# A sparse-attention and feed-forward kernel: another opening, block means by a selecting matrix, raw weights in the low parts' place

## The chip, the cores and the metric

The kernel runs on one core of one Trainium2 chip. Times are microseconds of device time of one execution, the median of several. One profiled execution gives the trace; there times count from the start of its span.

## The reference, cut to what matters

```python
# q, k, v: (2 batches, 8 heads, 768 positions, 64)
k_sum = k.reshape(B, H, nb, 32, D).max(axis=3)          # block maxima of keys, nb = 24
v_sum = v.reshape(B, H, nb, 32, D).mean(axis=3)         # block means of values
scores_l = scale * q @ k.T, kept where |i - j| < 16, else -1e9
scores_s = scale * q @ k_sum.T + np.log(32)
a = softmax(concatenate([scores_l, scores_s]))
attn = a @ concatenate([v, v_sum])
x = attn as (1536 tokens, 512)
h = maximum(maximum(x @ w1, x @ w2), x @ w3)            # 512 to 768 columns
x = h @ w_out                                           # the feed-forward's result
# then a second mixture of experts: each token with a positive skip score
# passes through one of 8 experts (512 to 1024 to 512) and is added to x
```

## The kernel before, in words

All data is fp32. Products of the feed-forward are made from three fp32r products, of high and low parts: a high part is a rounding copy on ScalarE, a low part is the difference on VectorE. So each weight piece (`w_hi`, `w_lo`) and each block of activations (`x_hi`, `x_lo`, `h_hi`, `h_lo`) is split once.

The kernel has three stretches: attention, the feed-forward, then routing and the experts. The first two are interleaved by an order written out by hand on every engine.

Attention has 24 steps. Step g takes a pair of heads and four tiles of 64 queries. The first twelve steps belong to batch 0 (pairs 0 to 3, each three times, in turn), the others to batch 1. On TensorE a step has three parts: `scores(g)` (windows of 96 keys and 24 block maxima), `turn_probs(g)` (four transposes of the normed probabilities) and `values(g)` (product with the value windows and block means). Between them VectorE scales, masks and takes the maximum (`mask_max`), ScalarE takes four exponentials with row sums (`exps`), VectorE inverts the sums (`invert`), GpSimd multiplies (`norm`), and ScalarE copies the turned probabilities out of PSUM. `x_high` and `x_low` split the result of a step. One PSUM tile holds the scores of one step, and one the values.

Keys of a pair come as `k_all`. VectorE takes the block maxima (`key_max`) and copies windows and maxima into `k_w` (`place_keys`), for all 12 tiles of the pair at once. The block means of values are made on GpSimd from `v_all` by five halving sums (`value_sums`), turned by TensorE (`turn_sums`) and placed by ScalarE (`place_sums`).

The feed-forward has 6 groups of 256 tokens, four steps' results each. A group has 20 units: units 0 to 17 are products of 12 matmuls (six hidden tiles, three weights each), units 18 and 19 are the down products, of 18 matmuls of 512 columns. The maximum over the three weights is taken by a copy on ScalarE (`h_a`) and two maxima on VectorE (`h_m`); `hidden_hi` and `hidden_lo` split it. Three PSUM banks turn among the units. Unit 18 needs hidden tile k at its k-th step of contraction. Between units of the next group, TensorE also transposes the group's result rows and makes logits of them (`tail`).

`step(g)` interleaves: from step 6 on (`FIRST`), five units ride in each step, split in three by `PARTS`. A step on TensorE is scores(g + 2), units, turn_probs(g), units, values(g - 1), units. Units that remain run behind step 23, so group 4 holds the last two attention steps and group 5 none.

The weights are 8 pieces of 768 KB: pieces 0 to 5 hold one hidden tile's three weights, 6 and 7 the down weights. A piece comes into one of two raw buffers (`raw_w`); ScalarE makes the high part and issues the load of the next piece, which waits until VectorE has taken the low part of the piece before. `SPLITS` says in which step which piece is split. All other loads are issued by the SP queue in a fixed order, each behind a wait for its buffer.

## Time and profile before

| | before |
|---|---|
| median of 3 runs | 536.09 us (535.78 to 537.84) |
| the profiled execution | 535.93 us, its span 534.1 us |
| TensorE busy | 465.2 us (87%) |
| VectorE busy | 209.0 us (39%) |
| ScalarE busy | 179.6 us (34%) |
| GpSimd busy | 79.9 us (15%) |
| mean granted TensorE clock | 0.952 of 2.4 GHz |

The shares are averages over the whole span. What an engine does in one stretch is read from the rows by stage, and which wait ends last there from the chain and the timeline.

### The profile page before, as it was taken

How to read it: one execution, taken by the hardware profiler on the slowest of the kernel's cores; microseconds unless marked ns; L12 is line 12 of the kernel's file. 1: busy time of each engine (PE TensorE's matmuls, PEld its weight loads, DVE VectorE, ACT ScalarE, POOL GpSimd, SP SyncE). 2: the span in 40 equal slices, each digit the busy share in tenths (PEclk: the TensorE clock that was granted, in tenths of full speed). 3: DMA queues.
4: the chain of work that ended last, by engine and by line, in shares of the span. 5: the costliest groups of instructions: out<-in, count | busy, mean ns of one | idle time of the engine just before them, and what ended most of it. 6: DMA issues, size and time to landing. Idle time of an engine off the chain costs nothing.

```text
span 534.1 us, 9695 instructions
## 1 busy us (share of the span) xinstructions
PE 465.2 (87%) x3409; PEld 401.6 (75%) x3410; DVE 209.0 (39%) x475; ACT 179.6 (34%) x461; POOL 79.9 (15%) x99
## 2 busy tenths in 40 slices
PE   1557868999999999999999951698999999999974
PEld 1337867899899899999999941476777777787753
DVE  5674457343333323412302237627422222222371
ACT  2585333443433243333111113427222222222360
POOL 2641003322010000010000000011111111111111
PEclk9988879999999999999999975799999999999998
DMA  8747431242130112020020024944611111111000
GB/s 262 254 135 243 139 110 56 56 135 76 29 105 26 39 45 97 16 80 1 14 80 1 2 79 178 360 152 147 216 50 39 39 39 39 39 39 35 22 15 2
DMA packets 20239, 46.64 MB, mean 87 GB/s; under 512 B 3580, under 2 KB 7164, under 8 KB 20208
## 3 DMA queue, kind: packets, MB, share of 16 engines
q1 hardware_dynamic: 16944, 35.25, 19.5%
q0 software_dynamic: 2400, 6.24, 3.5%
q10 hardware_dynamic: 864, 4.72, 2.6%
q8 instruction: 21, 0.34, 0.2%
q14 instruction: 10, 0.08, 0.1%
HBM read 37.86 MB, written 9.96 MB: 90 GB/s over the span
## 4 chain that ended last, share of the span: by engine, by line
PE 77%; DVE 6%; DMA 5%; issue 5%; ACT 3%; SPq 1%; DVEq 1%; POOL 1%; ACTq 0%; POOLq 0%
PE bank L497 29%; PE pair L613 14%; PE bank L603 12%; PE bank L512 9%; PE bank L446 2%; PE pair L416 2%; PE bank L595 2%; PE bank L434 2%; PE bank L539 2%; DMA raw_w<-ffn_w_dram 2%; DMA k_all<-k_all_dram 1%; DMA rows<-x_rows,index_next 1%; DMA e_raw<-experts_dram 1%; DVE e_lo L918 1%; ACT w_hi L668 1%
## 5 line engine op out<-in xcount | busy, mean ns | idle before, releaser
L497 PE MATMUL bank<-x_hi,w_hi 128*128 128x256 f32 x432 | 129.1, 299 | 10.1 <-DVE h_m L860 10.1
L497 PE MATMUL bank<-x_lo,w_hi 128*128 128x256 f32 x432 | 124.4, 288 | 0.0
L497 PE MATMUL bank<-x_hi,w_lo 128*128 128x256 f32 x432 | 124.3, 288 | 0.0
L497 PEld LDWEIGHTS bank<-x_hi,w_hi 128*128 128x128 f32 x432 | 85.0, 197 | 13.4 <-DVE h_m L860 10.5
L497 PEld LDWEIGHTS bank<-x_lo,w_hi 128*128 128x128 f32 x432 | 85.0, 197 | 0.1
L497 PEld LDWEIGHTS bank<-x_hi,w_lo 128*128 128x128 f32 x432 | 84.8, 196 | 0.0
L1142 POOL DMA_INDIRECT rows<-x_rows,index_next x16 | 16.5, 1032 | 244.7 <-DVE index_next L1067 155.9
L613 PE MATMUL pair<-e_hi,u_hi 128*128 128x512 f32 x112 | 48.3, 431 | 4.5 <-DVE u_lo L1064 3.5
L1064 DVE TENSOR_TENSOR u_lo<-bank,u_hi 128x512 fp32r<-128x512 f32 x28 | 19.3, 691 | 82.1 <-ACT u_hi L747 82.1
L603 PE MATMUL bank<-e_hi,r_hi 128*128 128x512 f32 x112 | 46.5, 415 | 3.7 <-DVE e_lo L918 2.1
L1108 POOL TENSOR_TENSOR probs<-probs,rowinv 128x480 f32<-128x480 f32 x24 | 25.6, 1067 | 160.2 <-DVE rowinv L817 160.2
L860 DVE TENSOR_TENSOR h_m<-h_a,bank 128x256 f32<-128x256 f32 x36 | 15.1, 421 | 76.1 <-PE bank L497 75.9
L603 PE MATMUL bank<-e_hi,r_lo 128*128 128x512 f32 x112 | 44.8, 400 | 0.0
L613 PE MATMUL pair<-e_hi,u_lo 128*128 128x512 f32 x112 | 44.5, 398 | 0.0
L603 PE MATMUL bank<-e_lo,r_hi 128*128 128x512 f32 x112 | 44.5, 397 | 0.0
L613 PE MATMUL pair<-e_lo,u_hi 128*128 128x512 f32 x112 | 44.4, 396 | 0.0
L701 ACT COPY h_a<-bank 128x256 f32<-128x256 f32 x36 | 13.3, 370 | 87.8 <-PE bank L497 81.0
L751 ACT ACTIVATE up<-bank 128x512 f32<-128x512 f32 x28 | 16.7, 598 | 68.0 <-PE bank L603 66.7
L647 ACT ACTIVATE probs<-probs,negmax 128x120 f32<-128x120 f32 x96 | 36.8, 391 | 8.2 <-DVE negmax L810 8.1
L613 PEld LDWEIGHTS pair<-e_hi,u_hi 128*128 128x128 f32 x112 | 21.4, 191 | 13.8 <-issue 6.0
L864 DVE TENSOR_TENSOR h_m<-h_m,bank 128x256 f32<-128x256 f32 x36 | 15.2, 421 | 40.8 <-PE bank L497 40.7
L757 ACT CAST e_hi<-e_raw 128x1024 fp32r<-128x1024 f32 x24 | 24.1, 1047 | 18.6 <-DMA e_raw<-experts_dram 16.2
(153 smaller groups left out, 750.4 us busy)
## 6 DMA issues: line engine op xcount, KB each, us to landing
e_raw<-experts_dram SPq DMA_DIRECT2D x24, 512.0 KB, 5.6
v_w<-v_dram SPq DMA_DIRECT2D x24, 192.0 KB, 2.5
raw_w<-ffn_w_dram ACTq DMA_DIRECT2D x6, 768.0 KB, 4.4
k_all<-k_all_dram SPq DMA_DIRECT2D x8, 400.0 KB, 4.3
q_t<-q_dram SPq DMA_DIRECT2D x24, 128.0 KB, 3.0
v_all<-v_all_dram SPq DMA_DIRECT2D x8, 384.0 KB, 6.2
x_rows<-y_rows SPq DMA_DIRECT2D x12, 256.0 KB, 2.3
out_dram<-y_rows SPq DMA_DIRECT2D x12, 256.0 KB, 2.3
```

Of the source, the lines that this page charges most:

```text
L497: mm = pe.matmul(ring_of(gr, n)[:, 0:GT], w_parts[a][:, f, (w * KD + k) * P:(w * KD + k + 1) * P], x_parts[c][:, gr % XS, k, :], start=i = ...
L512: mm = pe.matmul(ring_of(gr, UPS + t), h_parts[a][:, k, t * P:(t + 1) * P], w_parts[c][:, KF + k // 3, k % 3 * DM:(k % 3 + 1) * DM], start ...
L603: mm = pe.matmul(ps_up[half][:], (r_hi, r_lo)[a][:, k, :], (e_hi, e_lo)[c][:, k, half * 512:(half + 1) * 512], start=(k == 0 and a + c == ...
L613: mm = pe.matmul(ps_down[:], (u_hi, u_lo)[a][:, f, :], (e_hi, e_lo)[c][:, KD + f // 2, (f % 2) * DM:(f % 2 + 1) * DM], start=(f == 0 and a ...
L647: last = act.activation(probs[r][:, i, :], probs[r][:, i, :], ACT.Exp, bias=negmax[:, r, i:i + 1], accum_out=rowsum[:, r, i:i + 1])
L751: act.activation(up[:, half * 512:(half + 1) * 512], ps_up[half][:], ACT.Relu).then_inc(relu_done, 1)
L757: act.copy(e_hi[:, c, :], e_raw[:, c, :]).then_inc(e_hi_done, 1)
L860: dve.tensor_tensor(h_m[f % 2][:], h_a[:], ring_of(gr, n)[:, 0:GT], ALU.max).then_inc(h_ab_done, 1)
L864: dve.tensor_tensor(h_m[f % 2][:], h_m[f % 2][:], ring_of(gr, n)[:, 0:GT], ALU.max).then_inc(h_done, 1)
L1064: dve.tensor_tensor(at_, ps_up_t[half][:], hi, ALU.subtract).then_inc(u_lo_done, 1)
L1108: pool.tensor_tensor(probs[r][:], probs[r][:], rowinv[:, r, :].unsqueeze(2).to_broadcast([P, QUAD, KC]), ALU.mult).then_inc(normed, 1)
L1142: pool.indirect_dma_start(rows[:], None, x_rows, bass.IndirectOffsetOnAxis(ap=index_next[:, 0:1], axis=0), bounds_check=T - 1, oob_is_err= ...
```

## The change

- The feed-forward's units ride from step 4 on and not from step 6. Scores run one step ahead and not two, `values(g)` follows in its own step, and the exponentials and `x_high`/`x_low` move accordingly. In the fourth step of each group no unit stands between scores and `turn_probs`.
- Steps 0 to 3 are written out by hand ahead of the loop, on each engine. TensorE's list is in the diff. ScalarE: exps 0, exps 1, turned_probs 0, exps 2, turned_probs 1, exps 3, place_means 0 and 1, x_high 0, turned_probs 2, place_means 2, x_high 1, first_weights_high 0, place_means 3, turned_probs 3, x_high 2, first_weights_high 1, x_high 3, first_weights_high 2, exps 4. VectorE: key_max and place_keys 0 and 1, mask_max 0, key_max 2, place_keys 2, mask_max 1, invert 0, key_max 3, place_keys 3, mask_max 2, place_keys 4, invert 1, mask_max 3, place_keys 5, invert 2 and 3, x_low 0 and 1, first_weights_low 0, mask_max 4, x_low 2, first_weights_low 1, x_low 3, first_weights_low 2, invert 4.
- The block means of batch 0 are made by TensorE: six products of `v_sel` (1/32 where a value row belongs to a block) with value rows in their natural order (`v_nat`, three loads of 512 KB), and one copy per pair on ScalarE. Batch 1 keeps the halving sums, whose loads now wait for `vsum_placed`, as they lie where `v_nat` lay.
- `w_raw` holds all 8 raw pieces in the place of `w_lo`, and the low part is written over the raw one. All pieces are loaded by SP; piece 0 comes in three thirds, each split apart. Piece f + 1 is split during unit 3f of group 0, pieces 6 and 7 at units 15 and 17.
- `place_keys` works by step (4 tiles) with three buffers; queries have six buffers; each of batch 0's four `k_all` has a buffer of its own. The mask comes in two halves.
- SP's opening list: keys 0, query 0, mask half 0, keys 1, query 1, ident, keys 2, query 2, v_sel, value rows 0, keys 3, query 3, value rows 1 and 2, values 0 and 1, weights 0 first third, values 2, mask half 1, query 4, values 3, weights 0 second and last third, weights 1, query 5, weights 2, values 4, weights 3, query 6, values 5, weights 4, query 7, values 6, weights 5, values 7, weights 6 and 7. `load_values(g)` waits for value product g - 4 and `load_queries(g)` for scores g - 6.

```diff
-LEAD = 2
-RAW = 2
+THIRD = WCH // 3
+KWS = 3
+QS = 6
+VT = S // P
...
         w_hi = place("w_hi", [P, WPIECES, WCH], F32R)
+        at["w_raw"] = at["top"]
         w_lo = place("w_lo", [P, WPIECES, WCH], F32R)
+        w_raw = place("w_raw", [P, WPIECES, WCH], F32, "w_raw")
...
-        PARTS = (cut(0, 2, 4, 6), cut(6, 8, 10, 12), cut(12, 14, 16, 18), cut(18, 19, 19, 20))
+        PARTS = (cut(0, 2, 4, 6), cut(6, 8, 10, 12), cut(12, 14, 16, 18), cut(18, 18, 19, 20))
         NONE = ((), (), ())
-        FIRST = PPB + LEAD
-        KEY_MAX = {0: 2, 1: 3, 8: 4, 9: 5, 10: 6, 11: 7}
-        SUM_TURN = {0: 0, 1: 1, 2: 2, 3: 3, 10: 4, 11: 5, 12: 6, 13: 7}
-        SPLITS = {3: (0,), 4: (1,), 5: (2,), 6: (3, 4), 7: (5, 6), 8: (7,)}
+        FIRST = PPB
+        KEY_MAX = {2 * PPB + i: PPB + i for i in range(PPB)}
+        VALUE_SUMS = {2 * PPB + i: PPB + i for i in range(PPB)}
+        SUM_TURN = {2 * PPB + 1 + i: PPB + i for i in range(PPB)}
...
             def scores(g):
-                p, c = pair_of(g)
-                pe.wait_ge(k_placed, p + 1)
-                pe.wait_ge(q_in[g % RING], 16 * (g // RING + 1))
+                pe.wait_ge(k_placed, g + 1)
+                pe.wait_ge(q_in[g % QS], 16 * (g // QS + 1))
                 at_least(pe, masked, g)
                 for j in range(QUAD // 2):
                     for h, odd in ((0, 0), (1, 1), (0, 1), (1, 0)):
                         i = 2 * j + odd
                         mm = pe.matmul(ps_scores[odd * QT:(odd + 1) * QT, h, j * KC:(j + 1) * KC],
-                                       q_t[h * D:(h + 1) * D, g % RING, i, :],
-                                       k_w[h * D:(h + 1) * D, p % PPB, c * QUAD + i, :], start=True, stop=True)
+                                       q_t[h * D:(h + 1) * D, g % QS, i, :],
+                                       k_w[h * D:(h + 1) * D, g % KWS, i, :], start=True, stop=True)
                 mm.then_inc(scores_done, 1)
+            def sum_values(j):
+                if j % 2 == 0:
+                    pe.wait_ge(v_nat_in[j // 2], 16)
+                if j == 0:
+                    pe.wait_ge(v_sel_in, 16)
+                first = (VT - 1 - j) * QUAD
+                mm = pe.matmul(ps_sums, v_sel[:, first:first + KC], v_nat[:, j, :], start=j == 0, stop=j == VT - 1)
+                if j == VT - 1:
+                    mm.then_inc(v_nat_summed, 1)
...
                 gr, parts = ffn_of(g)
                 if g in SUM_TURN:
                     turn_sums(SUM_TURN[g], g)
-                if g + 2 < STEPS:
-                    scores(g + 2)
+                if g + 1 < STEPS:
+                    scores(g + 1)
                 for n in parts[0]:
                     unit(gr, n)
                 turn_probs(g)
                 for n in parts[1]:
                     unit(gr, n)
-                if g > 0:
-                    values(g - 1)
+                values(g)
                 for n in parts[2]:
                     unit(gr, n)
...
+            def weights_split(i):
+                if i > 0:
+                    pe.wait_ge(w_lo_done, by_vector(i))
...
             scores(0)
             scores(1)
+            scores(2)
+            sum_values(0)
+            sum_values(1)
             pe.wait_ge(ident_in, 16)
-            for g in range(STEPS):
+            turn_probs(0)
+            scores(3)
+            sum_values(2)
+            sum_values(3)
+            turn_probs(1)
+            sum_values(4)
+            sum_values(5)
+            values(0)
+            turn_probs(2)
+            values(1)
+            scores(4)
+            turn_probs(3)
+            values(2)
+            values(3)
+            for g in range(FIRST, STEPS):
                 step(g)
...
+            def place_means(p):
+                act.wait_ge(v_nat_summed, 1)
+                act.copy(v_w[KW:KC, p, :, :],
+                         ps_sums[KW:KC, p * P:(p + 1) * P].unsqueeze(1).to_broadcast([NSUM, QUAD, P])
+                         ).then_inc(vsum_placed, 1)
+            def first_weights_high(t):
+                act.wait_ge(first_w_in[t], 16)
+                act.copy(w_hi[:, 0, third(t)], raw_of(0)[:, third(t)]).then_inc(w_hi_done, 1)
             def weights_high(i):
-                act.wait_ge(raw_w_in[i % RAW], 16 * (i // RAW + 1))
-                act.copy(w_hi[:, i, :], raw_w[:, i % RAW, :]).then_inc(w_hi_done, 1)
-                if 2 <= i + 1 < WPIECES:
-                    load_raw(act, i + 1)
+                act.wait_ge(raw_w_in[i], 16)
+                act.copy(w_hi[:, i, :], raw_of(i)).then_inc(w_hi_done, 1)
+            def turned_probs(g):
+                act.wait_ge(probs_t_done, g + 1)
+                at_least(act, pv_done, g - 1)
+                act.copy(probs_t[g % 2][:], ps_probs_t[0:KC]).then_inc(probs_t_copied, 1)
             def step(g):
                 gr, parts = ffn_of(g)
                 if g in SUM_TURN:
                     place_sums(SUM_TURN[g])
-                if g > 1:
-                    x_high(g - 2)
+                for n in parts[0]:
+                    unit(gr, n)
                 if g + 1 < STEPS:
                     exps(g + 1)
-                for n in parts[0]:
-                    unit(gr, n)
-                act.wait_ge(probs_t_done, g + 1)
-                at_least(act, pv_done, g - 1)
-                act.copy(probs_t[g % 2][:], ps_probs_t[0:KC]).then_inc(probs_t_copied, 1)
-                for i in SPLITS.get(g, ()):
-                    weights_high(i)
+                turned_probs(g)
                 for n in parts[1]:
                     unit(gr, n)
-                if g == STEPS - 1:
-                    x_high(g - 1)
+                x_high(g)
                 for n in parts[2]:
                     unit(gr, n)
-                if g == STEPS - 1:
-                    x_high(g)
             def unit(gr, n):
                 f = n // 3
...
+                    if gr == 0 and f + 1 < KF:
+                        weights_high(f + 1)
+                if gr == 0 and n in (UPS - 3, UPS - 1):
+                    weights_high(KF + (n == UPS - 1))
                 if n in TURNS and gr > 0:
                 if n == UPS:
...
-            def place_keys(p):
-                if p >= PPB:
-                    dve.wait_ge(scores_done, 2 * PPB + p - PPB + 1)
-                keys = k_all[p % 2][:]
-                windows = bass.AP(tensor=keys.tensor, offset=keys.offset, ap=[keys.ap[0], [QT, TILES], [1, KW]])
-                dve.tensor_copy(k_w[:, p % PPB, :, 0:KW], windows)
+            def place_keys(g):
+                p, c = pair_of(g)
+                at_least(dve, scores_done, g - KWS + 1)
+                dve.wait_ge(k_all_in[p % PPB], 16 * (p // PPB + 1))
+                keys = k_all[p % PPB][:, c * QUAD * QT:]
+                windows = bass.AP(tensor=keys.tensor, offset=keys.offset, ap=[keys.ap[0], [QT, QUAD], [1, KW]])
+                dve.tensor_copy(k_w[:, g % KWS, :, 0:KW], windows)
                 dve.wait_ge(ksum_made, p + 1)
-                dve.tensor_copy(k_w[:, p % PPB, :, KW:KC],
-                                ksum[:, p, :].unsqueeze(1).to_broadcast([P, TILES, NSUM])).then_inc(k_placed, 1)
+                dve.tensor_copy(k_w[:, g % KWS, :, KW:KC],
+                                 ksum[:, p, :].unsqueeze(1).to_broadcast([P, QUAD, NSUM])).then_inc(k_placed, 1)
...
+            def first_weights_low(t):
+                dve.wait_ge(w_hi_done, t + 1)
+                dve.tensor_tensor(w_lo[:, 0, third(t)], raw_of(0)[:, third(t)], w_hi[:, 0, third(t)].bitcast(F32),
+                                  ALU.subtract).then_inc(w_lo_done, 1)
             def weights_low(i):
-                dve.wait_ge(w_hi_done, i + 1)
-                dve.tensor_tensor(w_lo[:, i, :], raw_w[:, i % RAW, :], w_hi[:, i, :].bitcast(F32), ALU.subtract
+                dve.wait_ge(w_hi_done, 3 + i)
+                dve.tensor_tensor(w_lo[:, i, :], raw_of(i), w_hi[:, i, :].bitcast(F32), ALU.subtract
                                   ).then_inc(w_lo_done, 1)
             def step(g):
                 gr, parts = ffn_of(g)
+                if g + 1 < STEPS:
+                    mask_max(g + 1)
+                for n in parts[0]:
+                    unit(gr, n)
                 if g in KEY_MAX:
                     key_max(KEY_MAX[g])
-                    place_keys(KEY_MAX[g])
                 if g + 2 < STEPS:
-                    mask_max(g + 2)
-                if g > 1:
-                    x_low(g - 2)
+                    place_keys(g + 2)
+                for n in parts[1]:
+                    unit(gr, n)
                 if g + 1 < STEPS:
                     invert(g + 1)
-                for i in SPLITS.get(g, ()):
-                    weights_low(i)
-                for n in parts[0]:
-                    unit(gr, n)
-                for n in parts[1]:
-                    unit(gr, n)
-                if g == STEPS - 1:
-                    x_low(g - 1)
+                x_low(g)
                 for n in parts[2]:
                     unit(gr, n)
-                if g == STEPS - 1:
-                    x_low(g)
             def unit(gr, n):
                 f = n // 3
+                if gr == 0 and n < UPS and n % 3 == 0 and 0 < f + 1 < KF:
+                    weights_low(f + 1)
+                if gr == 0 and n in (UPS - 3, UPS - 1):
...
-            value_sums(0)
-            norm(0)
-            for g in range(STEPS):
-                if g + 1 in SUM_TURN:
-                    value_sums(SUM_TURN[g + 1])
+            for g in range(FIRST + 1):
+                norm(g)
+            for g in range(FIRST, STEPS):
+                if g in VALUE_SUMS:
+                    value_sums(VALUE_SUMS[g])
...
+    v_sel = np.zeros((P, KC + (VT - 1) * QUAD), f)
+    v_sel[np.arange(P), KC - QUAD + np.arange(P) // BLOCK] = 1.0 / BLOCK
```

## Rows read from the trace of the kernel before

**Rows 1.** Stages; columns: length; busy PE, PEld, DVE, ACT, POOL; clock, DMA share, GB/s.
```profile
0.00:42.24 42.24, 19.35 (x253) 13.62 (x254) 26.15 (x50) 23.43 (x77) 19.49 (x32) 0.92 0.68 212
42.24:99.83 57.59, 46.80 (x385) 42.78 (x381) 30.82 (x53) 21.35 (x58) 10.73 (x13) 0.88 0.41 135
...
144.94:189.53 44.59, 44.59 (x425) 41.06 (x427) 14.72 (x39) 15.90 (x58) 4.04 (x4) 1.00 0.17 55
...
234.11:274.01 39.90, 39.90 (x335) 37.92 (x334) 9.20 (x25) 10.39 (x32) 0.99 (x1) 1.00 0.10 32
```

**Rows 2.** The chain from 144.5 to 190 us: start, length, what.
```profile
172.26 0.44 PE bank L434 x4
172.70 2.87 PE bank L497 x24
...
176.18 3.06 PE bank L497 x24
179.25 0.57 PE pair L416 x16
179.82 4.35 PE bank L512 x18
...
184.61 0.61 PE bank L446 x16
```

**Rows 3.** TensorE's waits from 40 to 257 us: total, times, longest.
```profile
PE bank L497 <- DVE h_m L860: 10.1, 3, 4.6
```

**Rows 4.** The chain from 42 to 100 us, ahead of unit 3 of group 0.
```profile
47.25 4.39 DMA raw_w<-ffn_w_dram
51.67 1.48 ACT w_hi L668
```

**Rows 5.** Busy time from 56 to 57 us; columns as in rows 1.
```profile
56.00:57.00 1.00, 1.00 (x7) 1.00 (x6) 0.00 (x0) 1.00 (x6) 0.00 (x0) 0.50 1.02 336
```

**Rows 6.** Busy time from 10 to 20 us; columns as in rows 1.
```profile
10.00:20.00 10.00, 3.65 (x37) 2.03 (x30) 7.30 (x14) 5.43 (x22) 7.22 (x13) 1.00 1.06 333
```

**Rows 7.** The chain from 0 to 60 us.
```profile
5.90 7.18 DMA k_all<-k_all_dram
...
29.17 1.62 ACT probs L647 x8
```

**Rows 8.** Timeline of the opening: start, length, engine, line, operation, idle before.
```profile
3.99 0.95 DVE L786 TENSOR_REDUCE ksum<-k_all 128x24 f32<-128x768 f32 x1 [3.87 <-DMA k_all<-k_all_dram]
...
4.86 0.75 DVE L794 COPY k_w<-k_all 128x1152 f32<-128x1152 f32 x1
...
5.53 0.30 DVE L796 COPY k_w<-ksum 128x288 f32<-128x288 f32 x1
...
5.88 1.08 PE L416 MATMUL pair<-k_w,q_t 64*64 64x120 f32 x16 [5.88 <-DVE k_w L796]
...
9.46 0.65 DVE L810 TENSOR_REDUCE negmax<-probs 128x4 f32<-128x480 f32 x1
...
24.68 0.73 PE L416 MATMUL pair<-k_w,q_t 64*64 64x120 f32 x16
...
24.79 0.59 ACT L662 ACTIVATE v_w<-bank 24x512 f32<-24x512 f32 x1 [0.87 <-PE bank L426]
...
25.40 0.37 ACT L656 CAST x_hi<-bank 128x256 fp32r<-128x256 f32 x1
...
26.75 0.41 DVE L822 TENSOR_TENSOR x_lo<-bank,x_hi 128x256 fp32r<-128x256 f32 x1
...
31.29 0.99 POOL L1108 TENSOR_TENSOR probs<-probs,rowinv 128x480 f32<-128x480 f32 x1 [2.51 <-DVE rowinv L817]
...
32.66 1.76 DVE L827 TENSOR_TENSOR w_lo<-raw_w,w_hi 128x1536 fp32r<-128x1536 f32 x1 [1.46 <-ACT w_hi L668]
...
36.16 1.12 PE L446 MATMUL bank<-probs_t,v_w 120*64 120x64 f32 x16 [3.18 <-DVE x_lo L822]
...
36.38 2.53 POOL L1108 TENSOR_TENSOR probs<-probs,rowinv 128x480 f32<-128x480 f32 x1 [4.11 <-DVE rowinv L817]
```

More of the change, by code:

```diff
@@ L116, in program @@
         rowinv = place("rowinv", [P, PROBS, QUAD])
-        at["rows"] = at["top"]
-        raw_w = place("raw_w", [P, RAW, WCH])
+        ROWS = at["rows"] = at["top"]
+        v_nat = place("v_nat", [P, VT, DM])
         y_rows = [place(f"y_rows{i}", [P, DM], F32, "rows") for i in range(TPG)]
         y_t = place("y_t", [P, KD, P], F32, "rows")
+        v_all = [place(f"v_all{i}", [P, S], F32, "rows") for i in range(2)]
         ones = place("ones", [P, P], BF16, "ffn")
@@ L316, in ring_of, with third, by_vector, raw_of @@
             return ps_ring[(UNITS * gr + n) % len(ps_ring)]
[L318 to L320 removed]
+        def third(t):
+            return slice(t * THIRD, (t + 1) * THIRD)
+        def by_vector(i):
+            return 3 + i
+        def raw_of(i):
+            return w_raw[:, i, :]
         @block.sync
@@ L385, in _ @@
+            for s in range(PPB, STEPS):
+                if s + PPB < STEPS:
+                    load_queries(s + PPB)
+                    load_values(s + PPB)
+                if s in (4, 5, 8, 9):
+                    load_all_values({4: 4, 5: 5, 8: 6, 9: 7}[s])
+                if 6 <= s < 6 + PPB:
+                    load_all_keys(s - 6 + PPB)
+                if s >= 8 and s % PPB == 0:
+                    store_rows((s - 8) // PPB)
             sp.wait_ge(x_lo_done, GQ)
@@ L723, in _ @@
             exps(0)
-            for g in range(STEPS):
+            exps(1)
+            turned_probs(0)
+            exps(2)
+            turned_probs(1)
+            exps(3)
+            place_means(0)
+            place_means(1)
+            x_high(0)
+            turned_probs(2)
+            place_means(2)
+            x_high(1)
+            first_weights_high(0)
+            place_means(3)
+            turned_probs(3)
+            x_high(2)
+            first_weights_high(1)
+            x_high(3)
+            first_weights_high(2)
+            exps(4)
+            for g in range(FIRST, STEPS):
                 step(g)
-            for n in range(PARTS[PPB - LEAD][0][0], UNITS):
-                unit(GROUPS - 2, n)
             gr = GROUPS - 1
```

166 lines of the change are left out of this document (102 added, 64 removed).

## The prediction

> **What bounds the kernel now.** I read the stages first, cut where the chain of waits shows a group of the feed-forward to begin and end [rows 1]. TensorE computes all six groups of 256 tokens. From the second group on it is busy in every microsecond, at 2.4 GHz: a group with four attention steps takes 44.59, the one with the last two of them 39.90. There only less TensorE work would help, and the change takes none away. The other part is the start: the first unit is issued at 42.24, TensorE having worked 19.35 us of those 42.24; and group 0 takes 57.59 from its first unit. Its own work comes from the steady chain [rows 2]: nine pairs of units at 2.87 (25.8), two down products at 4.35 less 0.19 (8.3), and inside them three scores at 0.57, four turns at 0.44 and four value products at 0.61 (5.9), with the 0.19 by which 3.06 exceeds 2.87 behind each of the scores and value products (1.3): 41.4. So 16.2 us of group 0 are loss. The waits name VectorE's `h_m` for 10.1 us of it, in three waits [rows 3]. The chain shows that the `h_m` operation only came last: behind it are `raw_w`'s transfer, 4.39, then ScalarE's high part (1.48) and VectorE's low part (1.76) [rows 4, 8]. Two raw buffers, refilled once a low part is taken, feed the weights too late. Most of the rest is the clock: after the longest wait, which ended at 55.3, TensorE runs at 1.2 GHz [rows 5].
>
> Behind the feed-forward nothing is touched, so I carry that stretch over. The gain is: (42.24 - new first unit) + 16.2 - new losses - added work behind the start. The last: the attention leads by four steps and not six, so the fifth group holds four steps of attention too: 44.59 - 39.90 = 4.7 us that before lay in the opening.
>
> **The opening, part by part.** Loads. The opening moves 333 GB/s between 10 and 20 us [rows 6]. The third `k_all` lands at 13.1 [rows 7], with 2.9 MB issued up to it. In the new order the SP queue puts 1.68 MB ahead of that tile's landing; 2.8 MB ahead of the fourth's; 4.0 to the last value rows; 4.65 to the first third of weights; 6.7 to query 5, which step 4's scores need, behind weights 1. With 0.32 MB per us from 2 us on, and 1.2 us lag (which gives the 13.1 within 0.8), these land at 8.5, 12.1, 15.7, 17.8 and 24.3. SP issues 25 loads in some 12 us before it first waits, so issuing is no bound. Weights 3 to 7 stand behind values 4 to 7, each of which waits for a value product; those come at 24 to 29 us, and the queue has weights 1 and 2 to move until 27. Weight 3 then lands near 30 and weight 7 near 42; ScalarE first wants weight 3 at about 43. The transfers leave the chain, and so do ScalarE's DMA issues.
>
> VectorE. Placing keys costs 0.75 + 0.30 per pair of 12 tiles [rows 8]. For 4 tiles I take a third and some fixed cost, 0.45 in all; 24 of them make 10.8 against 8.4, but each first one is 0.6 earlier, and later ones lie between units where VectorE is a third busy [rows 1]. With key maximum 0.95, mask and maximum 1.3 (two passes of 0.65), exponentials 1.6, inversion 0.35 and GpSimd's norm 0.99 [rows 7, 8] the new list runs: key maximum 0 from 4.0, placed 0 at 5.4; tile 1 in at 6.6, placed 1 at 8.0; mask 0 to 9.35; key maximum 2 and placing 2 to 10.8; mask 1 to 12.1, inversion 0 to 12.4, norm 0 to 13.5; tile 3 to 13.8; mask 2 to 15.1; placing 4 and inversion 1 to 15.9, norm 1 to 17. Scores 2 need placing 2 and mask 1's reading: 11.5 to 12.6. GpSimd's value sums no longer stand ahead of the norms.
>
> TensorE's new work: six products with `v_sel`, 512 columns, plain fp32. The trace has none. Lower bound: an fp32r product of 512 columns, 4.35/18 = 0.24 us [rows 2]. Upper: value products do 4 rounds of 64 fp32 columns in 0.61, 2.4 ns a column, so 1.22 us warm [rows 2] and 2.3 at 1.2 GHz (1.12 for the same products [rows 8]). I take the upper, since the value products have the data type and the long contraction of the new ones. When cold, scores took 1.08; at 24.68 they take 0.73, full speed coming with them, after TensorE had worked almost without a pause since 21.2 [rows 8]. In the new order it works so from 11.5 on, and I take the first product and a part of the second as cold. The Trainium skill (FP8 and Floating Point Precision, TensorE Precision Notes) says true fp32 makes four passes; by that a product is an estimated 4 x 0.24 = 0.96 warm and the whole time 1.5 to 2 us less, 517. The trace agrees in direction: fp32 columns cost 2.4 ns here, those of fp32r 0.47.
>
> Products 0 and 1 then end at 16.1, turn 0 and scores 3 at 17.2, products 2 and 3 at 19.6, turn 1 at 20.1, products 4 and 5 at 22.5. Behind that nothing can be overlapped: means of pair 0 on ScalarE (0.59), values 0 at 23.1, then for each of steps 0 to 3 high part 0.37, low part 0.41, next values 0.61 [rows 2, 8], with ScalarE's other means, copies of turned probabilities and a third of weights (0.5 to 0.6 each), and VectorE's mask 4 (1.3) ahead of low part 2. I get values 1 at 24.6, values 2 at 26.4, values 3 at 28.6, x_lo 3 at 30.05. First weight third is ready at 26.9, the second at 29. **First unit at 30.1**, 12.1 us earlier. Bounds: 28.0 with the cheap products (then ScalarE's exponentials of step 3 set the means); 38.8 with everything cold: six products at 2.3 and two turns and scores at 1.1 end at 29.7, and 7.6 + 1.5 follow.
>
> **New losses.** Group 0. Norm 4 is done at 33.3, turn 4 wanted at 33.1: 0.2. The split of piece f+1 starts only after the first unit of piece f: a copy like x_hi's 0.37 + high 1.48 + low 1.76 = 3.6 later. In between TensorE has two units (1.44 each [rows 2]) and a turn, 3.3, or two attention parts and more: every second piece costs 0.3, three times: 0.9.
>
> At the last step of a group the change turns the order round: TensorE now does scores, turn, then unit 18; ScalarE has `exps(g+1)` and the copy of turned probabilities ahead of `hidden_hi(5)`, which unit 18 needs at its sixth tile. With T the end of unit 17, unit 18 begins at T + 1.0 and wants hidden 5 at T + 4.45 (15 of its 18 products, 4.16 in all). Scores and mask/maximum give T + 2.1, exponentials T + 3.7, copy T + 4.2, high T + 4.6, low T + 5.0. That is 0.6 of stall in each of groups 1 to 3: 1.8 (group 4 has no next exponentials there). In group 0 VectorE is late itself: low parts 6 and 7 (1.7 each), inversion, x_lo and unit 16's maximum push unit 17's maximum to T + 2.9; hidden_lo 4, the mask, exponentials and copy follow, hidden_lo 5 at T + 7.5: 3.1 us. Such a pause is as long as the 3.18 after which the value products of 36.16 ran at half speed [rows 8]; half a chance of 1 us: 0.5.
>
> Sum of losses 0.2 + 0.9 + 1.8 + 3.1 + 0.5 = 6.5; bounds 1 (queue order hidden, no odd pieces) and 10 (clock drops in earnest). Norms beside low parts can take 2.53 and not 0.99 [rows 8]; here the norms have 3 us of slack, but in the last step, where the later stall covers it. The Trainium skill (SBUF — State Buffer, Who interferes with whom) has a vector operation with two SBUF inputs and a GpSimd one block each other in order of issue; by it low part 7 waits 0.3 for norm 7, and the time would be 0.3 longer.
>
> Total: 12.1 + 16.2 - 4.7 - 6.5 = 17.1 us gained. The profiled execution took 535.93 (its span 534.1 and 1.8 around it), so 518.8; the median is 0.16 above it: 519.
>
> **Rivals.**
> Unit 18 does not wait, as VectorE or ScalarE reach hidden 5 in time, and the products lie half way between their bounds (0.7 each, first unit 2 earlier): gain 12.1 + 2 + 16.2 - 4.7 - 2.5 = 23, 513. For it: before, groups 1 to 3 had no wait at all [rows 1]. Against: there the turn came behind unit 18, and its copy stood behind `hidden_hi(5)` and not ahead of it. Chance 0.17.
> TensorE cold through the opening, or the loads later than by rate: first unit 34 to 38.8, losses 8: gain 8.2 + 16.2 - 4.7 - 8 = 11.7, or 3.4 in place of the 8.2, 6.9; 524 to 529. For it: it was cold until 24.7 before [rows 8], and a queue of 5 MB ahead of query 5 is deeper than any in the trace. Against: products fill the gaps. Chance 0.17.
> The change moves the weights' wait only: pieces 3 to 7 are issued behind `load_values`, and if these waits came late (15 us), group 0 would lose its 16.2 again: 12.1 - 4.7 - 2.5, some 531; where also the opening stayed, no change, 536. Chance 0.04.
> Slower: unit 18's wait for hidden 5, in four groups. Without losses the gain is 23.6, so it decides from 5.9 us a group against my 0.6 and 3.1. Only a clock that falls in the wait and stays at 1.2 GHz through both down products (8.3 more) could bring it: 4 x 8.9 = 35.6, and the time 548. The trace shows a low clock only after waits of 3 us and more [rows 5, 8]. Chance 0.03.
> My own course: 0.59, with its own range 515.5 to 523.
>
> **How the numbers follow.** A measurement of this kernel can tell about 0.5% (2.7 us) from no change. The range takes the two neighbours in to most of their width: 512 to 527.5; outside lie the extremes. Faster by over 0.5%: 0.59 + 0.17 + 0.17 + 0.02 = 0.95; within: 0.02; slower: 0.03.
>
> **What would show it.** Right: first unit at 28 to 33 us, six products of 0.9 to 1.3 us with the last ending near 22; group 0 in 44 to 48 us and no wait on a weight transfer; groups 1 to 3 at 45.2 each instead of 44.6; in unit 18 a gap with `h_lo` as releaser, near 3 us once and 0.6 thrice; fifth group 44.6. Wrong: products of 2 us and more at 1.2 GHz past 20 us; query 5 or key tiles as releaser in the opening; low parts that hold up whole units.

## The result and the profile after

| | before | changed |
|---|---|---|
| median, timed side by side | 535.93 us (534.63 to 537.84) | 521.81 us (519.40 to 522.00) |
| the profiled execution (span) | 535.93 (534.1) | 521.78 (520.0) |
| TensorE busy | 465.2 us | 466.0 us |
| mean granted TensorE clock | 0.952 | 0.966 |

The ratio is 0.972 [0.968, 0.976]: 14.1 us faster, where 17.1 were forecast; 521.8 stands 2.8 us above the predicted 519. The stages, cut as in [rows 1]: opening, groups 0, 1 and 2, the fifth group, the stretch behind the feed-forward:

```profile
0.00:30.18 30.18, 17.14 (x188) 10.17 (x189) 16.37 (x41) 15.01 (x50) 4.34 (x9) 1.00 0.95 303
30.18:80.34 50.16, 45.78 (x384) 40.73 (x387) 28.71 (x57) 25.14 (x69) 7.38 (x10) 0.93 0.41 130
80.34:126.31 45.97, 45.39 (x428) 41.23 (x431) 20.11 (x51) 17.77 (x62) 11.29 (x19) 1.00 0.29 88
126.31:171.67 45.36, 44.77 (x424) 40.90 (x427) 16.68 (x47) 16.32 (x59) 3.95 (x4) 1.00 0.16 53
217.06:260.89 43.83, 43.83 (x407) 40.83 (x407) 14.42 (x39) 14.29 (x50) 2.96 (x3) 1.00 0.05 17
299.06:520.00 220.94, 186.18 (x893) 146.85 (x893) 87.84 (x202) 67.00 (x98) 30.92 (x30) 0.93 0.25 88
```

The 14.1 us between the two spans are made up of these: first unit 42.24 to 30.18, 12.06; group 0 57.59 to 50.16, 7.43; groups 1 to 3 longer by 2.44 in all (45.97, 45.36 and 45.39 now); the fifth group longer by 3.93 (39.90 to 43.83); and 0.97 behind the feed-forward, which nothing in the change touches (two loads there took 0.5 less and 0.9 more; the rest of it is not settled).

**The opening.** The chain of waits (start, length, what):

```profile
11.71 1.08 PE pair L462 x16
12.79 3.70 PE bank L474 x4
...
17.64 1.91 PE bank L474 x4
...
20.61 1.51 ACT probs L723 x8
...
22.15 0.59 ACT v_w L744
...
22.78 0.69 PE bank L503 x16
...
28.17 0.34 DVE x_lo L924
...
28.65 0.70 PE bank L503 x16
...
30.25 4.64 PE bank L559 x24
```

A selecting product is recorded as two instructions, so the first pair took 3.70, 1.85 each, and the second 1.91, 0.95 each. By its length the first pair ran at half speed. The profile's granted clock does not show that: it reads 1.00 in every microsecond from 12 to 17 here, as it does in [rows 6] of the kernel before. So that TensorE was at 1.2 GHz early in the opening, here and in the prediction, is inferred from lengths alone (16 score products took 1.08 at 11.7 and 0.57 at 17.1). The price is 0.95 and not the 1.22 that the sum took. The Trainium skill (FP8 and Floating Point Precision, TensorE Precision Notes) has four passes for true fp32; four of 0.24 are 0.96, and the trace agrees. The last product ended at 21.7 (predicted 22.5). But the products do not then set the means: ScalarE's exponentials of step 3 run until 22.12, and the means start at 22.15. Four value products started at 22.78, 24.5, 26.3 and 28.65.

**Group 0.** TensorE's waits from 20 to 310 us (total, times, longest). [rows 3] is gone; in its place stands the predicted one on `h_lo`:

```profile
PE bank L574 <- DVE h_lo L979: 4.0, 4, 2.4
...
PE bank L503 <- DVE x_lo L924: 2.1, 2, 1.7
PE bank L491 <- POOL probs L1232: 1.1, 1, 1.1
...
PE bank L559 <- DVE w_lo L934: 0.8, 2, 0.4
```

How it comes about at unit 18 is read from the chain:

```profile
67.83 0.41 DVE h_m L969
68.24 0.34 DVE h_lo L979
68.57 0.58 DVE probs L907
...
69.17 0.66 DVE negmax L912
...
70.16 1.32 ACT probs L723 x7
71.48 0.47 ACT probs_t L759
71.95 0.32 ACT h_hi L800
...
72.29 0.44 DVE h_lo L979
...
72.86 0.93 PE bank L574 x3
73.80 0.61 PE bank L503 x16
74.41 5.93 PE bank L574 x18
```

Hidden tile 5's maximum had been ready since 68.24. Its two splits stand behind the next step's mask, maximum and exponentials in the written order. The second down product then took 5.93 in place of 4.35 [rows 2], most of it at 1.2 GHz (granted clock 0.84 from 74 to 75, 0.50 from 75 to 78). The same happened at the first units: 24 matmuls took 4.64, where they took 3.14 in a version whose clock did not fall there (e8 below). The windows (columns as in [rows 1]):

```profile
30.00:31.00 1.00, 0.75 (x3) 0.75 (x4) 0.89 (x2) 1.00 (x6) 0.00 (x0) 0.66 0.99 336
31.00:32.00 1.00, 1.00 (x7) 1.00 (x6) 0.17 (x1) 0.78 (x5) 0.00 (x0) 0.50 1.08 348
...
75.00:76.00 1.00, 1.00 (x4) 0.72 (x3) 0.29 (x1) 0.00 (x0) 0.84 (x3) 0.50 0.56 123
```

### The profile page after: what moved, and what is told of

Read it like the earlier page. It is cut to its first block, busy times and chain, and to the rows that moved or that the text cites. A ratio compares the mean times of both kernels' runs of the same rounds, so it can differ in the third digit from the quotient of the medians.

```text
span 520.0 us, 9745 instructions
## 1 busy us (share of the span) xinstructions
PE 466.0 (90%) x3417; PEld 397.7 (76%) x3418; DVE 209.0 (40%) x509; ACT 178.8 (34%) x463; POOL 64.8 (12%) x79
## 4 chain that ended last, share of the span: by engine, by line
PE 77%; DVE 8%; ACT 5%; issue 5%; DMA 3%; DVEq 1%; SPq 1%; ACTq 0%; POOL 0%; POOLq 0%
PE bank L559 30%; PE pair L689 15%; PE bank L679 12%; PE bank L574 8%; PE bank L503 3%; PE bank L671 2%; PE pair L462 2%; PE bank L601 2%; PE bank L491 1%; DMA e_raw<-experts_dram 1%; ACT probs L723 1%; DMA rows<-x_rows,index_next 1%; DVE e_lo L1042 1%; PE bank L474 1%; DVE w_lo L934 1%
## 5 line engine op out<-in xcount | busy, mean ns | idle before, releaser
L559 PE MATMUL bank<-x_hi,w_lo 128*128 128x256 f32 x432 | 122.8, 284 | 0.0
L559 PE MATMUL bank<-x_lo,w_hi 128*128 128x256 f32 x432 | 122.7, 284 | 0.0
L559 PEld LDWEIGHTS bank<-x_hi,w_hi 128*128 128x128 f32 x432 | 83.2, 193 | 5.2 <-issue 2.2
L559 PEld LDWEIGHTS bank<-x_lo,w_hi 128*128 128x128 f32 x432 | 83.4, 193 | 0.0
L559 PEld LDWEIGHTS bank<-x_hi,w_lo 128*128 128x128 f32 x432 | 83.2, 193 | 0.0
L1232 POOL TENSOR_TENSOR probs<-probs,rowinv 128x480 f32<-128x480 f32 x24 | 23.7, 987 | 208.6 <-DVE rowinv L919 208.6
L679 PE MATMUL bank<-e_lo,r_hi 128*128 128x512 f32 x112 | 44.6, 398 | 0.0
L1267 POOL DMA_INDIRECT rows<-x_rows,index_next x16 | 16.5, 1031 | 220.3 <-DVE index_next L1191 155.2
L965 DVE TENSOR_TENSOR h_m<-h_a,bank 128x256 f32<-128x256 f32 x36 | 15.1, 420 | 50.1 <-PE bank L559 50.1
L574 PE MATMUL bank<-w_hi,h_hi 128*128 128x512 f32 x72 | 30.2, 419 | 4.0 <-DVE h_lo L979 4.0
```

Source lines behind the costliest of these rows:

```text
L559: mm = pe.matmul(ring_of(gr, n)[:, 0:GT], w_parts[a][:, f, (w * KD + k) * P:(w * KD + k + 1) * P], x_parts[c][:, gr % XS, k, :], start=i = ...
L574: mm = pe.matmul(ring_of(gr, UPS + t), h_parts[a][:, k, t * P:(t + 1) * P], w_parts[c][:, KF + k // 3, k % 3 * DM:(k % 3 + 1) * DM], start ...
L679: mm = pe.matmul(ps_up[half][:], (r_hi, r_lo)[a][:, k, :], (e_hi, e_lo)[c][:, k, half * 512:(half + 1) * 512], start=(k == 0 and a + c == ...
L965: dve.tensor_tensor(h_m[f % 2][:], h_a[:], ring_of(gr, n)[:, 0:GT], ALU.max).then_inc(h_ab_done, 1)
L1232: pool.tensor_tensor(probs[r][:], probs[r][:], rowinv[:, r, :].unsqueeze(2).to_broadcast([P, QUAD, KC]), ALU.mult).then_inc(normed, 1)
L1267: pool.indirect_dma_start(rows[:], None, x_rows, bass.IndirectOffsetOnAxis(ap=index_next[:, 0:1], axis=0), bounds_check=T - 1, oob_is_err= ...
```

## The experiments

My theory: raw weights, the opening and the order at unit 18 are three separate matters. The first two gain, the last loses, and the low clock at 30 us comes of the idle time ahead of it. Rival theories: the weights alone give most of the gain; the selecting products are the price of the opening; the low clock is independent of the gap. Ratios are to the kernel before, timed on the same chip.

| run | median us | ratio, 95% | first unit | group 0 |
|---|---|---|---|---|
| before | 535.93 | 1 | 42.24 | 57.59 |
| changed | 521.81 | 0.972 [0.968, 0.976] | 30.18 | 50.16 |
| e1 before, weights raw | 534.05 | 0.993 [0.990, 0.996] | 47.00 | 49.50 |
| e7 the same, issued later | 533.22 | 0.992 [0.989, 0.995] | 44.94 | 51.36 |
| e9 the same, six query buffers | 531.90 | 0.991 [0.988, 0.993] | 42.58 | 51.42 |
| e5 changed again | 521.70 | 0.971 [0.968, 0.973] | 30.09 | 50.1 |
| e3 one selecting product of six | 522.22 | 0.973 [0.970, 0.976] | 29.57 | 47.3 |
| e10 selecting products twice | 526.69 | 0.979 [0.976, 0.983] | 36.06 | 50.1 |
| e4 unread products in the gaps | 519.23 | 0.967 [0.964, 0.970] | 30.41 | 50.3 |
| e2 hidden 5 first | 518.01 | 0.965 [0.961, 0.968] | 30.00 | 46.36 |
| e6 e2 with earlier splits | 513.05 | 0.956 [0.953, 0.959] | 30.48 | 43.68 |
| e8 e6 with e4's products | 511.55 | 0.952 [0.949, 0.955] | 30.58 | 42.36 |

The last two columns come from one profiled execution each; there a low clock falls or not (below), so they are read beside the medians.

### e1: the kernel before with all raw pieces in the low parts' place

```diff
         w_hi = place("w_hi", [P, WPIECES, WCH], F32R)
+        at["w_raw"] = at["top"]
         w_lo = place("w_lo", [P, WPIECES, WCH], F32R)
+        w_raw = place("w_raw", [P, WPIECES, WCH], F32, "w_raw")
...
-            at_least(eng, w_lo_done, piece - RAW + 1)
-            eng.dma_start(raw_w[:, piece % RAW, :], dram["ffn_w"][piece]).then_inc(raw_w_in[piece % RAW], 16)
+            eng.dma_start(w_raw[:, piece, :], dram["ffn_w"][piece]).then_inc(raw_w_in[piece], 16)
...
                     load_values(s + RING)
+                if s + 2 < WPIECES:
+                    load_raw(sp, s + 2)
...
```

> The kernel before, with only the weight feed of the change: eight raw pieces in the place of the low parts, pieces 2 to 7 issued by SP in steps 0 to 5 instead of by ScalarE; order of all else, GpSimd's value sums and the lead of six steps stay. If the 16.2 us that group 0 lost were all the feed's, as the prediction summed them, group 0 takes 42 to 46 us and the time is 520 to 524. My theory now, after looking at the chain again: the transfers (4.4 twice) go, but the splits of two pieces in one step still stand ahead of the unit's maximum on VectorE, so the waits of 4.6 and 4.5 shrink to some 2.4 each and the low clock behind them (1.7 and 2.0) goes: 8 us less, 527 to 529, first unit still at 42.2. Rival: the waits on the weights were only covered by others, and nothing changes (535 to 536).

Group 0 gained 8.1 us as I expected, and the opening lost 4.8 of them, which I did not; the time is 534.05 and not 527 to 529. Its chain, then the waits from 20 us on, then the windows of the opening and of one microsecond in it:

```profile
25.40 0.48 PE pair L419 x13
25.88 5.57 DMA q_t<-q_dram
...
38.70 1.12 PE bank L449 x16
```

```profile
PE bank L500 <- DVE h_m L861: 5.7, 3, 2.4
...
PE pair L419 <- DMA q_t<-q_dram: 2.7, 1, 2.7
```

```profile
0.00:47.00 47.00, 21.05 (x252) 14.84 (x253) 28.42 (x50) 25.49 (x84) 17.96 (x32) 0.84 0.76 242
38.00:39.00 1.00, 0.30 (x6) 0.33 (x8) 0.81 (x4) 1.00 (x1) 0.08 (x1) 0.50 1.04 433
```

A query of a later step was issued behind a raw piece on the SP queue and landed 5.57 us later. TensorE waited, and the granted clock fell to 0.50 at 32.2, to come back at 49.3; in the kernel before it was low from 35.2 to 45.4. The value product at 38.70 took 1.12, as its like at 36.16 did before [rows 8]; what is new is the longer stretch at 1.2 GHz. The opening's mean clock is 0.84; before it was 0.92 [rows 1]. So the cheaper weights were paid with a later query and the low clock behind it. `h_m` still waits for 5.7: the splits themselves, 1.4 and 1.8, remain in the middle of a piece.

### e7 and e9: pieces issued later, then queries fetched earlier

```diff
-                if s + 2 < WPIECES:
-                    load_raw(sp, s + 2)
+                for i in {3: (2,), 4: (3, 4), 5: (5, 6), 6: (7,)}.get(s, ()):
+                    load_raw(sp, i)
...
```

e9 has beside this `QS = 6` buffers for `q_t`, as the changed kernel has, with queries 4 and 5 in the opening list.

> The kernel before with only the weight feed of the change, as in the first experiment, but pieces 2 to 7 issued in SP's steps 3 to 6 so that no query stands behind them in the opening. There the first unit came 4.8 us later, with 2.7 us of waiting on queries in the chain, while group 0 had lost 8 us of its 16. If the queries behind 768 KB pieces were the cause, the first unit is back at 42 to 43 and the time is 8 us under before: ratio 0.984 to 0.987. If the opening is late for another reason (1.2 GHz by chance), it stays at 0.990 to 0.995.

> As the seventh experiment (the kernel before with only the weight feed of the change), and six query buffers as the changed kernel has: queries 4 and 5 are loaded in SP's opening list, and each later one two steps ahead of where the kernel before loads it. In the seventh the first unit came at 44.9, as query 8 stood behind piece 2 in the queue and scores 8 waited 3.3 us. If that is all that gave the feed's gain back, the first unit is at 42 or earlier, group 0 loses 8 us less than its 16, and the ratio is 0.983 to 0.987. If the waits only move to another load (values, keys) it stays near 0.992.

Issuing later wins back 2.1 us of the opening, and group 0 is 1.9 longer than in e1. That is not waiting (`h_m` stands at 5.7 in both) but clock: 24 matmuls from 68.80 took 4.55 where those of e1 from 70.47 took 3.14, and the first 24 took 4.46 and not 4.06. The ratio, 0.992, is not the 0.984 to 0.987 that I expected if no query were late, but one still was. SP issued query 8 right behind piece 2, and the scores that need it came late. The profile names no releaser for them but "issue"; that it was the query I read from SP's order, and e9 bears it out. From the timeline of e7:

```profile
37.00 1.38 SPq L321 DMA_DIRECT2D w_raw<-ffn_w_dram  x1
...
38.43 0.43 SPq L328 DMA_DIRECT2D q_t<-q_dram  x1
...
43.93 1.08 PE L419 MATMUL pair<-k_w,q_t 64*64 64x120 f32 x16 [3.31 <-issue]
```

With six query buffers no query is late, and the first unit is where it was (42.58, before 42.24). Group 0 is 6.2 shorter, and the median 5.0 us lower (536.89 to 531.90), where I expected 7 to 9. With the pieces issued so late, one transfer still stands in the chain, and `h_m` is waited for 7.0 in place of e1's 5.7:

```profile
38.01 5.59 DMA w_raw<-ffn_w_dram
```

So the weight feed alone is worth 5.0 in the best form that was tried, and 8.1 in group 0 where e1 issued it early. By that some 5 to 8 of the change's 14.1 are the weights, and the rest is the opening less what it costs later. This is an estimate: no run has the changed opening with the old weight feed, so the rival that most of the gain is weights is weakened and not refuted.

### e3 and e10: the selecting products, one and twelve

```diff
+                if j < VT - 1:
+                    return
...
+                for i in range(VT // 2):
+                    pe.wait_ge(v_nat_in[i], 16)
...
-                mm = pe.matmul(ps_sums, v_sel[:, first:first + KC], v_nat[:, j, :], start=j == 0, stop=j == VT - 1)
+                mm = pe.matmul(ps_sums, v_sel[:, first:first + KC], v_nat[:, j, :], start=True, stop=True)
```

```diff
+                pe.matmul(bank[7][0:KC], v_sel[:, first:first + KC], v_nat[:, j, :], start=True, stop=True)
                 mm = pe.matmul(ps_sums, v_sel[:, first:first + KC], v_nat[:, j, :], start=j == 0, stop=j == VT - 1)
```

e3 leaves five of six selecting products out, so its block means cover one tile of values only.

> The changed kernel with one of the six products of the selecting matrix; the other five are left out, so the means hold only the last rows' share. If the products set the opening, as the prediction had it (4.7 us of them cold, 4.8 warm), the first unit comes 2 to 3 us earlier, but TensorE, less busy, may stay at 1.2 GHz all through the opening, which gives 1 to 2 us back: 518.5 to 520.5. If the exponentials of step 3 set it alone, the first unit stays at 30 and the time within 0.5 us of 521.8. If the low clock weighs more than the products, slower: 522.5 to 524.

> The changed kernel with each of the six selecting products made twice, the second time into a free bank that nobody reads. The sum took the products as on the path. The trace of the changed kernel has them at 1.85 us (two, at 1.2 GHz) and 0.95 (four); with five left out the first unit came 0.7 earlier only. So doubled they should cost: all six on the path, 5.7 to 7.5 us later; my theory now: the first two fill idle time up to norm 0 and the rest up to the exponentials of step 3, of which 1 to 2 us is slack, so the first unit comes 3 to 5 us later than 30.1 and the time is 524 to 527. Rival: off the path, within 1 us of 521.8.

Taking some 6 us of TensorE's work out moved the first unit 0.6 forward and the median not at all. From e3's timeline:

```profile
21.20 1.12 PE L504 MATMUL bank<-probs_t,v_w 120*64 120x64 f32 x16 [1.09 <-ACT v_w L745]
...
27.96 0.69 PE L504 MATMUL bank<-probs_t,v_w 120*64 120x64 f32 x16 [1.16 <-DVE x_lo L925]
```

The first value product starts 1.6 earlier than in the changed kernel, but until 25.4 value products and turns take 1.1 each and not 0.6 to 0.7, by their length at half speed, and more than half of the lead is gone by the last value product (27.96 against 28.65). The time fits the second of the expectations, exponentials alone, and not the 518.5 to 520.5 of the first. Adding as much work moved the first unit back by 5.9, more than the 3 to 5 that I expected (median 5.0 above that of e5, 4.7 by the two ratios). So the products fill time that is idle without them, up to just about their own length: they stand at the edge of the path, with hardly any slack behind them. That they are the opening's price has fallen: without them it costs the same, in part because TensorE is then slower for longer.

### e4 and e5: gaps filled, and the changed kernel once more

```diff
+            def keep_busy(columns):
+                for n in columns:
+                    pe.matmul(bank[7][0:KC, 0:n], v_sel[:, 0:KC], v_nat[:, 0, 0:n], start=True, stop=True)
...
             sum_values(5)
+            keep_busy((448,))
             values(0)
...
             values(2)
+            keep_busy((512, 384))
             values(3)
```

> The changed kernel with three further products of the selecting matrix into a free bank (448 columns ahead of values 0, 512 and 384 ahead of values 3), whose results nobody reads: they fill the two longest idle times of TensorE in the opening, 1.1 and 1.7 us. If the clock fell at 30.3 because of the idle time at 27 to 28.6, the first 24 matmuls of group 0 take 2.9 instead of 4.6 us and the time is 520, 1.8 less. If it falls for another reason the time stays within 0.4 us of 521.8 or is up to 0.5 longer.

> The changed kernel unaltered, as the anchor on this chip: ratio to before 0.972 to 0.975. It also says whether the low clock at the start of group 0 (24 matmuls in 4.6 us) is there in each execution: in two of the three variants profiled so far it was absent with nothing done about it. If it is a matter of chance, the executions spread over some 2 us and this profile may show it or not; if it belongs to the kernel, it shows again.

e5 comes out at 0.971, just under the 0.972 to 0.975 expected, and its low clock at the start of group 0 is there again. In e4, with the gap of 1.7 us ahead of values 3 filled, no low clock followed at 30 us; the median is 2.5 below e5's, 1.9 by the ratios (0.967 [0.964, 0.970] beside 0.971 [0.968, 0.973]). These two intervals overlap, so the medians alone do not show the gain, and e4's profile has the other low clock, behind unit 18's wait (18 matmuls in 6.16). e8 over e6, the same edit, tells it better (below).

### e2: hidden tile 5 split first

```diff
# ScalarE, step(g)
                 for n in parts[0]:
                     unit(gr, n)
+                if UPS in parts[1]:
+                    hidden_hi(gr, KF - 1)
                 if g + 1 < STEPS:
                     exps(g + 1)
...
# VectorE, step(g)
+                if UPS in parts[1]:
+                    hidden_lo(gr, KF - 1)
                 if g + 1 < STEPS:
                     mask_max(g + 1)
...
```

The same two calls at unit 18 stay for the last group only.

> The changed kernel, with hidden_hi(5) ahead of exps(g+1) on ScalarE and hidden_lo(5) ahead of mask_max(g+1) on VectorE in the fourth step of each group. If unit 18 waits for hidden tile 5 because it is queued behind the exponentials, the four gaps with h_lo as releaser (2.4, 0.5, 0.5, 0.6) go, with them the 1.6 of low clock in the down products of group 0, and groups 1 to 3 fall from 45.4 to 44.6: 5 to 6.5 us less, 515.5 to 517. Rival: h_lo is only the last of several (bank, norm, split of piece 7), the gap stays under another name and the time stays within 1 us of 521.8. Second rival: the mask comes 1 us later and turns of the next step wait: 1 to 2 us of the gain given back.

```profile
30.00:76.36 46.36, 42.63 (x384) 38.20 (x387) 28.79 (x56) 25.05 (x69) 7.39 (x10) 1.00 0.41 134
76.36:121.66 45.30, 45.10 (x428) 41.32 (x431) 20.21 (x51) 17.85 (x62) 11.29 (x19) 1.00 0.28 89
121.66:166.27 44.61, 44.61 (x427) 41.08 (x430) 16.78 (x47) 16.46 (x60) 3.95 (x4) 1.00 0.16 54
166.27:210.80 44.53, 44.53 (x428) 40.99 (x428) 16.84 (x47) 15.91 (x59) 3.94 (x4) 1.00 0.20 64
```

```profile
PE bank L503 <- ACT probs_t L759: 1.7, 1, 1.7
```

The wait on `h_lo` is gone from the list of waits, and groups 1 to 3 are shorter by 0.7, 0.8 and 0.9, back at 44.6 and 44.5 for the last two. The median is 3.7 below e5's (3.2 by the ratios), less than the 5 to 6.5 that I expected. Group 0's 3.8 in this profile holds the low clock at the first units too, which did not come here. Less 1.5 for that, the order is worth 2.3 in groups 1 to 3 and 2.3 in group 0. In group 0 that is less than the 2.4 of wait and 1.6 of low clock that went, since the rival named beforehand came in part: the copy of turned probabilities is now late, and the value product waits 1.7 for it.

### e6 and e8: earlier splits, then both

```diff
                 if n < UPS and n % 3 == 0:
+                    if gr == 0:
+                        weights_high(f + 1)
+                        if n == UPS - 3:
+                            weights_high(f + 2)
                     at_least(act, h_ab_done, KF * gr + f)
                     act.wait_ge(unit_done, UNITS * gr + n + 1)
                     act.copy(h_a[:], ring_of(gr, n)[:, 0:GT]).then_inc(h_a_done, 1)
-                    if gr == 0 and f + 1 < KF:
-                        weights_high(f + 1)
...
-                if gr == 0 and n in (UPS - 3, UPS - 1):
-                    weights_high(KF + (n == UPS - 1))
...
```

The low part of piece 7 moves from unit 17 to unit 16. e8 adds e4's three products.

> The changed kernel with hidden tile 5 first (as in the second experiment), and the weights split earlier: ScalarE makes the high part of piece f+1 ahead of the copy of unit 3f instead of behind it, pieces 6 and 7 both at unit 15, VectorE takes low part 7 at unit 16 instead of 17. What was left of group 0's loss there was 0.2 + 0.4 + 0.4 for low parts, 1.1 for norm 7 and 1.7 for the copy of turned probabilities 7: if these come of the late splits, group 0 takes 42.5 to 43.5 us instead of 46.4, and the time is 3 to 4 us under that of the second experiment, ratio 0.957 to 0.960. Rival: ScalarE, now making 1.5 us copies ahead of each unit's copy, holds the bank and the maxima up, and gives all of it back.

> As the sixth experiment, with the three unread products in TensorE's idle times of the opening. If the clock falls by chance at the first unit, this takes 0.5 to 1 us off the median and narrows the spread; if it does not matter, the same time as the sixth within 0.5 us.

First e6, then e8, the whole of group 0 and the microsecond from 31 to 32:

```profile
30.48:74.16 43.68, 43.14 (x384) 39.53 (x388) 29.31 (x56) 25.07 (x69) 7.38 (x10) 0.96 0.46 146
31.00:32.00 1.00, 1.00 (x7) 1.00 (x6) 0.21 (x1) 1.00 (x7) 0.00 (x0) 0.50 0.98 344
```

```profile
30.58:72.94 42.36, 41.79 (x384) 38.08 (x387) 29.13 (x56) 24.96 (x69) 7.38 (x10) 1.00 0.47 151
31.00:32.00 1.00, 1.00 (x10) 1.00 (x9) 0.31 (x1) 1.00 (x6) 0.00 (x0) 1.00 0.96 356
```

The waits on `w_lo` and on the norm are both gone, and the wait for turned probabilities fell from 1.7 to 0.5. Against e2 the median is 5.0 lower (4.7 by the ratios), where 3 to 4 were expected; the rival that ScalarE would give it back has fallen. The 43.68 holds a low clock at the first units (24 matmuls in 4.62; in e8 in 3.14). The 1.3 us by which e8's group 0 is shorter is near the 1.5 by which its median is lower (0.5 to 1 was expected). Both ran on the same chip, five executions each, and the slowest of e8 (511.77) is below the fastest of e6 (512.26), though the intervals, [0.953, 0.959] and [0.949, 0.955], overlap a little. At 42.36 the group stands 1 us above its 41.4 of own work. e8 is the fastest version here: 511.55, 4.8% below the kernel before, and 10 us below the change.

## Why the prediction was right, and where not

The sum by its own terms, in us gained, against the profile:

| term | predicted | measured |
|---|---|---|
| first unit earlier | 12.1 | 12.06 |
| group 0 | 16.2 - 4.7 = 11.5 | 7.43 |
| groups 1 to 3, unit 18 waits | -1.8 | -2.44 |
| fifth group holds four steps | -4.7 | -3.93 |
| behind the feed-forward | 0 | 0.97 |
| sum | 17.1 | 14.1 |

- **The opening** came out right for partly other reasons, and that its term fits to 0.1 is luck. The products were 1.85 and 0.95, not 2.3 and 1.22, but both of a pair had the long duration, where I had one and a part of the next, and behind them the exponentials of step 3 took the path over. I had named that as what binds with cheap products, with the first unit then at 28.0. This was too low by 2: values 0 started 0.3 sooner than in my list, and values 1 to 3 on its times.
- **The transfers** left the path as predicted. Weight pieces took up to 14 us from issue to landing and no wait names one. e1 and e7 show that this is not free of itself: the same pieces in the older list made a query late by 3 us. The change's six query buffers hide them, a part that I had passed over at no cost and without naming what it covers; e9 shows it at work.
- **Group 0** is the mis-sized term: 46.1 predicted, 50.2 measured. The wait for hidden tile 5 was predicted at 3.1 and took 2.4, by the chain forecast (mask, exponentials, copy, high, low). Not in the sum were 1.5 for the low clock at the first units; 1.1 for a wait on norm 7, which I had thought to be covered by that stall; and 1.1 more of low clock behind it (1.6 against the 0.5 put in for half a chance). The waits on odd pieces were 0.4, not 0.3 each. About 1.2 us in stretches of under 0.3 was not followed; 0.3 of it is in the first 24 matmuls, which take 3.14 and not 2.87 at full clock too (e8).
- **The clock step** is what failed in kind: "The trace shows a low clock only after waits of 3 us and more". That was wrong of that very trace. Behind the feed-forward of the kernel before, TensorE waited 2.7 for ScalarE until 344.41, and the granted clock was 0.50 from 346 to 349; at 315.0 it fell with no wait of over 0.7 close before it. Here TensorE idled for 1.69 and slowed down 1.7 later:

```profile
28.65 0.69 PE L503 MATMUL bank<-probs_t,v_w 120*64 120x64 f32 x16 [1.69 <-DVE x_lo L924]
```

- **Groups 1 to 3**: 2.44 against 1.8. e2 takes back 2.3 by the order alone, so the mechanism is shown, at 0.8 a group in place of 0.6, of which 0.5 is the wait on `h_lo` itself.
- **The fifth group** holds four steps but three scores, since scores run one step ahead: 0.57 + 0.19 too many in my 4.7, and 44.59 - 0.76 is the measured 43.83.
- **The norm beside a low part.** The timeline has both at work at 65.8:

```profile
65.30 0.99 POOL L1232 TENSOR_TENSOR probs<-probs,rowinv 128x480 f32<-128x480 f32 x1 [10.58 <-DVE rowinv L919]
...
65.78 2.13 DVE L934 TENSOR_TENSOR w_lo<-w_raw,w_hi 128x1536 fp32r<-128x1536 f32 x1
```

The low part took 2.13 in place of 1.76 [rows 8], 0.37 longer. By the Trainium skill (SBUF — State Buffer, Who interferes with whom) the later of the two waits for the earlier, and the trace agrees in size with the 0.3 forecast from it. The norm stayed at 0.99 here. In [rows 8] it was the norm that took 2.53, and there a low part had started just ahead of it, at 36.30.

- **The total** is nearer than its parts. Against the sum, group 0 lost 4.1 more and groups 1 to 3 lost 0.6 more; the fifth group lost 0.8 less, and 1.0 came from behind the feed-forward, where nothing was forecast.

Of the rivals, that the wait at unit 18 does not come was wrong; the slower one was right in its mechanism and far from its price (2.4 and three of 0.5 against the 5.9 a group from which it decides). TensorE did not stay slow through the opening: by their length its instructions were slow until 16.5 only. Key tile 1 landed at 7.1, where the list had 6.6, and stands in the chain; after it no load does, and no wait names a weight transfer, so the other two did not come either.

## What to carry to other kernels

Where work is moved a step, write out each engine's list at the seam and ask for what the next TensorE unit waits; one line put ahead of another (hidden tile 5's split ahead of the next exponentials) was worth a quarter as much here as the whole change. A large load put early on a queue is paid by the small loads behind it, so give these more buffers first. A gap in TensorE's work costs its own length and, at times, nearly as much again in low clock behind it (here 1.7, and 1.2 to 1.5); filler products in the gaps cost hardly anything (e4's first unit at 30.41, the changed kernel's at 30.18).

## What was not expected of the hardware

After the gap of 1.7 us ahead of values 3, the clock fell to 1.2 GHz, 1.0 to 1.9 us behind the gap's end, in four of the five profiles that have the gap (the changed kernel, e5, e6, e10; not in e2) and in neither of the two that filled it (e4, e8); in e3 the gap is 1.2 and the clock did not fall. When it fell, it cost 1.2 to 1.5 us. In or behind the wait of 2.4 at unit 18 it fell in four of five profiles too (the changed kernel, e4, e5, e10; not in e3). So programs that are alike at this place fall on one side or the other, and what decides it these runs do not tell. With so few profiles the count alone could be chance; that filling the gap helps rests on e8 against e6. The spread is smaller where the gaps are filled: 518.9 to 523.4 for the changed kernel in e5, 510.2 to 511.8 for e8, which has those gaps filled and the wait at unit 18 gone. A small load (a query) right behind a 768 KB one on the same queue landed 5.6 us after its issue in e1, where the quickest query of the same stretch of e7 took 2.4.
